# Splitting the sum of squares into two fp32r halves for quarters two to four

## What is computed

```python
# 1: attention with a decaying state, 2 x 8 heads, 768 steps, head size 48
state = alpha[:, :, t, :, None] * state + einsum('bhd,bhe->bhde', k[:, :, t], v[:, :, t])
y[:, :, t] = einsum('bhd,bhde->bhe', q[:, :, t], state)
# 2: normalisation, then a gated layer, 384 -> 1536 -> 384
rms = sqrt(mean(x * x, axis=-1, keepdims=True) + 1e-06)
xn = x / rms * rms_g
g = xn @ w_gate
x = (g * (1 / (1 + exp(-g)))) * (xn @ w_val) @ w_out
# 3: four experts, 384 -> 1024 -> 384, summed by weight
p = domain_probs / (domain_probs.sum(-1, keepdims=True) + 1e-09)
out += p[:, e:e + 1] * (maximum(x @ w1[e], 0.0) @ w2[e])      # e = 0..3
```

## Time and profile before

| | us |
|---|---|
| median of 3 runs | 683.29 |
| lowest, highest | 682.52, 683.31 |
| the profiled execution | 682.79 |
| its span | 681.07 |
| PE busy | 673.6 |
| DVE busy | 469.8 |
| ACT busy | 266.8 |
| POOL busy | 326.8 |

### The profile page before, as it was taken

One profiled execution on the slowest core, in us unless ns is written; L12 is line 12 of the kernel. 1 busy time (PEld: TensorE's weight loads), 2 busy tenths in 40 slices (PEclk: granted clock), 3 DMA queues, 4 the chain that ended last, 5 costly groups with the idle time before them and its releaser, 6 DMA issues.

```text
span 681.1 us, 10689 instructions
## 1 busy us (share of the span) xinstructions
PE 673.6 (99%) x3915; PEld 625.9 (92%) x3915; DVE 469.8 (69%) x839; ACT 266.8 (39%) x485; POOL 326.8 (48%) x416
## 2 busy tenths in 40 slices
PE   8999999999999999999999999999999999999998
PEld 7799999999999999998999999999999999999997
DVE  6866648674676544029976977796778678867885
ACT  4525543233422352237533443343344344434430
POOL 3579661111111118870677448645854585468100
PEclk9999999999999999999999999999999999999999
DMA  9996465006411001000020110011011101100003
GB/s 153 175 229 159 108 94 81 10 8 88 77 34 47 1 1 47 0 24 0 10 85 2 48 46 29 20 46 48 11 37 48 47 0 47 47 24 1 24 0 140
DMA packets 91911, 35.67 MB, mean 52 GB/s; under 512 B 73552, under 2 KB 91344, under 8 KB 91856
## 3 DMA queue, kind: packets, MB, share of 16 engines
q1 hardware_dynamic: 91408, 34.96, 23.1%
q10 hardware_dynamic: 448, 0.00, 0.0%
HBM read 32.00 MB, written 2.36 MB: 50 GB/s over the span
## 4 chain that ended last, share of the span: by engine, by line
PE 91%; SPq 4%; DMA 2%; POOL 1%; issue 1%; DVE 0%; ACT 0%; POOLq 0%
PE out_ps L1467 13%; PE out_ps L1468 13%; PE out_ps L1469 13%; PE hid_ps L1460 7%; PE hid_ps L1462 7%; PE hid_ps L1461 7%; PE at_ps L1719 5%; PE at_ps L1718 5%; PE at_ps L1717 5%; SPq L492 3%; PE hid_ps L1718 2%; PE hid_ps L1719 2%; PE hid_ps L1717 2%; PE at_ps L1556 1%; PE at_ps L1596 1%; PE out_ps L1718 1%
## 5 line engine op out<-in xcount | busy, mean ns | idle before, releaser
L1343 DVE SCALAR_TENSOR_TENSOR x<-out_ps,prob,x 128x384 f32<-128x384 f32 x180 | 110.3, 613 | 57.6 <-PE out_ps L1469 57.6
L1468 PE MATMUL out_ps<-early_r,late_r 128*128 128x384 f32 x384 | 129.4, 337 | 0.0
L1469 PE MATMUL out_ps<-early_r,late_r 128*128 128x384 f32 x384 | 129.3, 337 | 0.0
L1467 PE MATMUL out_ps<-early_r,late_r 128*128 128x384 f32 x384 | 129.0, 336 | 0.0
L738 POOL TENSOR_TENSOR hid_lo<-act_sb,hid_hi 128x384 fp32r<-128x384 f32 x44 | 44.7, 1016 | 152.4 <-ACT hid_hi L965 152.4
L1015 ACT COPY late<-at_ps 128x512 f32<-128x512 f32 x105 | 61.9, 589 | 101.7 <-PE at_ps L1719 98.6
L1467 PEld LDWEIGHTS out_ps<-early_r,late_r 128*128 128x128 f32 x384 | 72.1, 188 | 6.1 <-DVE x L1343 0.2
L1468 PEld LDWEIGHTS out_ps<-early_r,late_r 128*128 128x128 f32 x384 | 72.0, 188 | 5.6
L1309 DVE TENSOR_TENSOR act_sb<-hid_ps,act_sb 128x384 f32<-128x384 f32 x48 | 26.0, 541 | 72.5 <-PE hid_ps L1462 71.9
L1469 PEld LDWEIGHTS out_ps<-early_r,late_r 128*128 128x128 f32 x384 | 72.1, 188 | 0.0
L754 POOL TENSOR_TENSOR early<-stage 128x128 f32<-128x128 f32 x15 | 7.0, 465 | 102.0 <-PE at_ps L1719 102.0
(11 more groups left out here) (300 smaller groups left out, 1607.0 us busy)
## 6 DMA issues: line engine op xcount, KB each, us to landing
stage<-in_moe_w_dram SPq DMA_DIRECT2D x32, 384.0 KB, 3.6
stage<-in_moe_w_out_dram SPq DMA_DIRECT2D x4, 576.0 KB, 5.2
out_dram<-x SPq DMA_DIRECT2D x12, 192.0 KB, 1.9
stage<-in_moe_w_gate_dram SPq DMA_DIRECT2D x8, 216.0 KB, 3.9
stage<-in_moe_w_val_dram SPq DMA_DIRECT2D x8, 216.0 KB, 4.1
v_tm<-in_v_dram SPq DMA_DIRECT2D x9, 192.0 KB, 4.1
x<-in_alpha_dram SPq DMA_DIRECT2D x6, 288.0 KB, 4.6
a_tm<-in_alpha_dram SPq DMA_DIRECT2D x31, 48.0 KB, 2.3
```

The source lines that it names most:

```text
L1343: dve.scalar_tensor_tensor(out=a, in0=part, scalar=p, in1=a, op0=ALU.mult, op1=ALU.add).then_inc(s_acc, 1)
L1467: pe.matmul(dst, ah, bh, start=first, stop=False)
L1468: pe.matmul(dst, ah, bl, start=False, stop=False)
L1469: return pe.matmul(dst, al, bh, start=False, stop=last)
```

## The change

For quarters two to four the sum of squares is split like other operands. ACT copies the sum with rounding to fp32r (step NH, at place 24), DVE subtracts that from the sum (step NJ, at place 25), and PE multiplies both halves with ones_r, an fp32r matrix of ones, into one bank. PE waits for the upper half ahead of the first product and for the lower half ahead of the second. ones_r is copied from ones by DVE in step FF. The halves lie in sq_split, which takes the same memory as x_nrm; its tiles 1 and 2 are those that N has added up. Quarter one is left as it is.

```diff
--- before.py
+++ after.py
@@ -59,6 +59,7 @@
         stage = sb("stage", [P, 2, KT * TQ])
         ident = sb("ident", [P, P])
         ones = sb("ones", [P, P])
+        ones_r = sb("ones_r", [P, P], F32R)
         gcol = sb("gcol", [P, KT])
         consts = sb("consts", [P, 3])
         zero = sb("zero", [P, 1])
@@ -106,6 +107,9 @@
         causal = sb("causal", [P, TQ], U8, stack=reg_a)
         x_last = sb("x_last", [P, TQ], stack=reg_a)
         x_raw = sb("x_raw", [P, KT, TQ], stack=reg_a)
+        reg_s = ExitStack()
+        sq_split = sb("sq_split", [P, KT, TQ], F32R, reg_s)
+        reg_s.close()
         x_nrm = sb("x_nrm", [P, KT, TQ], stack=reg_a)
         rms = sb("rms", [P, TQ], stack=reg_a)
         reg_a.close()
@@ -266,6 +270,7 @@
         s_hole = sem("s_hole")
         s_sq_redo = [sem(f"s_sq_redo{i}") for i in range(NQ)]
         s_sq, s_sqsum, s_ss, s_rms = sem("s_sq"), sem("s_sqsum"), sem("s_ss"), sem("s_rms")
+        s_sqh, s_sql = sem("s_sqh"), sem("s_sql")
         s_rinv = sem("s_rinv")
         s_xn, s_xh, s_xl = sem("s_xn"), sem("s_xh"), sem("s_xl")
         s_g, s_vv = sem("s_g"), sem("s_vv")
@@ -424,6 +429,8 @@
         for place in AT.values():
             place.sort(key=lambda step: step[0] != "Y")
         AT[STEP * NP].append(("N", 0))
+        AT[STEP * NP].append(("NH", 0))
+        AT.setdefault(STEP * NP + 1, []).append(("NJ", 0))
         AT.setdefault(STEP * NP + 3, []).append(("SS", 0))
         AT.setdefault(STEP * NP + 4, []).append(("R", 0))
         AT.setdefault(STEP * NP + 6, []).append(("X", 0))
@@ -930,6 +937,9 @@
                             squares(j, s_sq_redo[i])
                         act.wait_ge(s_sq_redo[i], KT)
                     act.sem_inc(s_sq, KT if i else KT + 1)
+                elif name == "NH":
+                    act.wait_ge(s_sqsum, i)
+                    act.copy(sq_split[:, 1, :], x_nrm[:, 0, :]).then_inc(s_sqh, 1)
                 elif name == "SS":
                     act.wait_ge(s_ss, i + 1)
                     act.activation(rms[:, :], at_ps[1][:, :], ACT.Abs_reciprocal_sqrt, bias=consts[:, 0:1],
@@ -1149,6 +1159,7 @@
                 u = NP * i + f
                 if name == "FF":
                     own(dve.tensor_scalar(first_fits[:, :], excess_sum[:, :], 0.0, None, ALU.is_le))
+                    own(dve.tensor_copy(ones_r[:, :], ones[:, :]))
                 elif name == "T":
                     dec, k_dm, q_dm, _, _, banks, _ = own_of(i, f)
                     if i >= BY_DVE:
@@ -1256,6 +1267,10 @@
                         own_done()
                     dve.tensor_tensor(x_nrm[:, 0, :], x_nrm[:, 0, :], x_nrm[:, KT - 1, :], ALU.add
                                       ).then_inc(s_sqsum, 1)
+                elif name == "NJ":
+                    dve.wait_ge(s_sqh, i)
+                    dve.tensor_tensor(sq_split[:, 2, :], x_nrm[:, 0, :], sq_split[:, 1, :].bitcast(F32), ALU.subtract
+                                      ).then_inc(s_sql, 1)
                 elif name == "R":
                     dve.wait_ge(s_rms, i + 1)
                     if i == 0:
@@ -1605,10 +1620,12 @@
                               ).then_inc(s_exsum, 1)
                 elif name == "SS":
                     if i:
-                        pe.wait_ge(s_sqsum, i)
+                        pe.wait_ge(s_sqh, i)
                         if i == 1:
                             pe.wait_ge(s_wild, 2)
-                        mm = pe.matmul(at_ps[1][:, :], ones[:, :], x_nrm[:, 0, :], start=True, stop=True)
+                        pe.matmul(at_ps[1][:, :], ones_r[:, :], sq_split[:, 1, :], start=True, stop=False)
+                        pe.wait_ge(s_sql, i)
+                        mm = pe.matmul(at_ps[1][:, :], ones_r[:, :], sq_split[:, 2, :], start=False, stop=True)
                     else:
                         for n, j in enumerate(FIRST_ORDER):
                             if n == 0:
```

## The result

| | before | after |
|---|---|---|
| median (us) | 683.25 (22 runs) | 682.24 (22 runs) |
| lowest, highest | 682.30, 684.99 | 681.18, 683.28 |
| profiled execution | 682.79 | 682.10 |
| its span | 681.07 | 680.4 |

The ratio is 0.9983, with a 95% interval from 0.9977 to 0.9989. By the medians that is 1.0 us less, by the interval between 0.8 and 1.6. Forecast were 0.9 us less, and a time of 682.4.

What follows compares the result with a forecast made beforehand. PE, busy 99% of the span, was taken to bound the kernel. The terms -1.94 + 1.04 + 0 (ACT) + 0 (DVE) + 0 (stall) gave -0.90 us, from 683.29 to 682.4 us; range 681.5 to 683.7.

Steps and rivals of the forecast that it cites:

- PE sheds 0.90 us: On PE in quarters two to four, three plain fp32 products (1.94 us) give way to six fp32r products (1.04 us).
- ACT hides the copy: The added 0.51 us copy on ACT delays the hid_hi cast 0.1 us at most and costs PE nothing.
- DVE hides the subtraction with 0.9 us to spare: The added 0.55 us subtraction on DVE ends 0.9 us before PE needs the lower half, so it costs nothing.
- rival 2: Lower half late at second product: 683.29-0.90+3x(L-0.9) us, L the subtraction's extra lateness; chance 0.06, including unseen causes.
- The 684.2 and 687.4 us: Times if table loads precede the added ACT copy: 684.2 with one load and one back, 687.4 with two loads ahead.
- ones_r costs 0.2 us, hidden: The single 128x128 copy on DVE in step FF takes 0.2 us, within 0.54 us of DVE idle time.
- The stall of quarter one moves along: PE's 0.28 us stall for hid_hi at quarter one's end stays that long, as the DVE work moves with PE.
- The sum has no other term: Beyond PE's -1.94 + 1.04, the ACT, DVE and stall terms are 0, giving -0.90 us in all.

Runs made afterwards that it cites:

- the three kernels with a late lower half: The changed kernel with the subtraction done two, three and five times in a row, each waiting for the last: 683.77, 685.70 and 692.76 us.
- the kernel with nothing removed: The changed kernel with all added work kept, but PE multiplying the unsplit sum by the plain fp32 product as before: 683.19 us, ratio 0.9997.

## Why the prediction was right

- **PE sheds 0.90 us.** Right. The three places shed 0.88 us in the profile after, and eight-fold both prices came out: 0.645 and 0.177 us, where the sum had 0.645 and 0.173. By the rule that the prediction takes from the Trainium skill's page "FP8 and Floating Point Precision", section "TensorE Precision Notes", a pair is half of a plain product, 0.32 us. Eight pairs would then take 2.6 us; they took 2.83, 0.354 a pair, and three single pairs shed 0.88 and not 0.97. The medians of the whole program don't tell the two figures apart.
- **ACT hides the copy.** Right: 0.52 us, no table load at line 942. The hid_hi cast behind it started at 167.94, 0.03 us after DVE's product was ready, where it was 0.04 before.
- **DVE hides the subtraction with 0.9 us to spare.** Right in the size (0.94 in the profile; 0.95 from the three kernels with a late lower half). The price of missing the margin, in rival 2, held only for short waits. With latenesses of 1.38 and 1.97 us, 3 x (L - 0.9) is 1.4 and 3.2 us; the medians gave 1.4 and 3.3, the profiled executions 1.7 and 3.5 on PE, with the 0.1 us behind each wait. With 3.16 us it is 6.8, and the median gave 10.4: the price left out the clock, about 1.5 us more wherever it fell. The 684.2 and 687.4 us of that rival weren't tried. The later expectations took 0.6 to 0.8 us for a step of DVE wherever it falls, while one beside POOL's hid_lo takes 1.35. That didn't bear on the forecast, as the one subtraction ends just as hid_lo begins (168.53 us in quarter three). If it fell on hid_lo it would take 0.8 us longer, and of the 0.95 us of margin about 0.15 would be left.
- **ones_r costs 0.2 us, hidden.** The size was wrong: 0.92 us, beyond my upper bound of 0.55. It ran past its cover of 0.54 us and set DVE's next product back by about 0.24 us. Hidden it was all the same: moving it away gained nothing that the median shows (0.9983 both times).
- **The stall of quarter one moves along.** Right: 0.46 us from start to start before and after, in the kernel with nothing removed as well.
- **The sum has no other term.** That was wrong, though it didn't spoil the forecast. The program's end got shorter too. Waits of SP at the end, before and after:

```profile
SPq L44 <- DMA out_dram<-x: 1.9, 1, 1.9
```

```profile
SPq L44 <- DMA out_dram<-x: 1.5, 1, 1.5
```

From the start of PE's last product to the end it is 3.69 and 3.70 us in the two kernels made from the one before (before, and eight plain products), and 3.29 to 3.30 in the twelve profiles of kernels made from the changed one, the one that keeps the plain product among them. So it isn't the product. What it is, the two added semaphores, the place of data in SBUF behind the added tile, or the layout of the program, stays open; it wasn't tried. With it the sum is 0.88 + 0.40 = 1.28 us less, with 0.08 lost on the way. That leaves 1.2 us; the measured 1.0 us (0.8 to 1.6) holds that and the forecast alike, so the hit to 0.1 us is in part luck.

What blurs the rest lies ahead of quarter two's SS. The 0.52 us by which the changed kernel was behind there came in three places, near 12, 39 and 52 us. The changed kernel run again had gained 0.17 us at the first, lost 1.0 at the second and gained 0.5 at the third, against its own first profile. The largest of them is a wait of PE for the load of q in quarter one: the time from the product before it to its start was 0.18 to 1.6 us in the profiled executions, with and without the change. The same place in the timelines of PE, the kernel before and the changed one run again:

```profile
39.19 0.55 PE L1540 MATMUL at_ps<-ident,q_tm 128*128 128x128 f32 x3
```

```profile
40.34 0.55 PE L1555 MATMUL at_ps<-ident,q_tm 128*128 128x128 f32 x3 [1.04 <-DMA q_tm<-in_q_dram]
```

That is why two profiled executions can't be compared by their spans here, and why distances behind 98 us were used.

## What to carry to other kernels

Where one engine is full, an edit is worth what it takes off that engine's queue, from start to start; a row's duration says 0.33 us for a product that costs 0.17. If a gain is near the scatter, repeat the disputed instruction until it isn't. Work put beside a full engine is free as long as it ends before the full engine asks for it: write down that margin, and look at what the engines beside it are doing at that moment, because it may cost double there.

## What the runs showed of the hardware

- DVE steps whose inputs and output all lie in SBUF took longer beside a TENSOR_TENSOR of POOL: a copy of 128x128 took 0.92 us (0.23 at the program's start, where POOL set up constants), a multiplication 0.97, a subtraction of 128x384 1.34 to 1.35 in place of 0.56 in all nine places where it began beside hid_lo. The copy and the multiplication ended 0.1 us behind POOL's instruction. V's product, which has one input in PSUM, ran 0.54 us beside the next of these POOL instructions. The Trainium skill, "GPSIMD Engine Reference", section "Key points", says that GpSimd shares its SBUF interfaces with VectorE, with contention for DVE instructions that have two SBUF inputs or run in a 2-port perf mode. The rows of the multiplication and the subtraction, with two inputs, agree with it; in which mode the copy ran no row shows.
- The kernel before has such a place too, at 305 us, and there the rows of both engines are longer: POOL's addition takes 0.66 us in place of 0.45, DVE's subtraction 0.67 in place of 0.56. Timelines of POOL and DVE:

```profile
304.67 0.45 POOL L766 TENSOR_TENSOR early<-early,stage 128x128 f32<-128x128 f32 x1
305.20 0.66 POOL L768 TENSOR_TENSOR early<-early,stage 128x128 f32<-128x128 f32 x1
304.87 0.67 DVE L1313 TENSOR_TENSOR hid_lo<-act_sb,hid_hi 128x384 fp32r<-128x384 f32 x1 [0.58 <-ACT hid_hi L965]
```

- Not every such step is held up. A RECIPROCAL of 128x384, with one input in SBUF, took 2.55 us where it began beside hid_lo, and the same elsewhere. In the changed kernel, POOL and DVE:

```profile
52.28 1.02 POOL L745 TENSOR_TENSOR hid_lo<-act_sb,hid_hi 128x384 fp32r<-128x384 f32 x1
52.89 2.55 DVE L1182 RECIPROCAL idec<-dec 128x384 f32<-128x384 f32 x1
```

- A wait of PE of 2.2 us between dense products was followed by 3.4 us at a granted clock of 0.50 in the three quarters of one execution, beginning 0.1 to 0.8 us after it resumed; the mean clocks of three more executions fit two quarters of three. Waits of 1.0 us, in the three quarters of one profiled execution, were not followed by it.
- The first product behind a wait of PE of 0.4 to 1.1 us started 0.28 us after the one that waited, in place of 0.17.
- The wait for the last output transfer was 0.4 us shorter in the programs made from the changed kernel (twelve against two); the cause is open.
